# Batch 1's first softmax turned by VectorE and carried to the key partitions through DRAM

## The reference

```python
def sm_attn(qq, kk, vv):
    s = scale * np.matmul(qq, kk.transpose(0, 1, 3, 2))
    s = s - np.max(s, axis=-1, keepdims=True)
    a = np.exp(s)
    a = a / (np.sum(a, axis=-1, keepdims=True) + 1e-09)
    return np.matmul(a, vv)
p_packed = sm_attn(p, k, v)
out = sm_attn(q, p_packed, p_packed)
```

## Time and profile before

| | |
|---|---|
| median of 3 runs | 1526.66 us |
| lowest and highest | 1525.93, 1527.21 us |
| the profiled execution, its own time | 1526.87 us |
| its span | 1525.0 us |
| granted TensorE clock | 1.000 |
| PE busy | 1514.4 us, 99% |
| VectorE, ScalarE, GpSimd busy | 48%, 29%, 13% |

### The profile page before, as it was taken

The page is one execution under the profiler, slowest core; times in us unless marked ns, Lnnn a source line. Parts: engine busy times, 40 slices in busy tenths (PEclk is TensorE's granted clock), DMA queues, the critical chain, the costliest instruction groups (busy, mean ns, idle before and its releaser), DMA issues.

```text
span 1525.0 us, 23354 instructions
## 1 busy us (share of the span) xinstructions
PE 1514.4 (99%) x9430; PEld 1258.7 (83%) x9430; DVE 726.0 (48%) x1234; ACT 444.6 (29%) x789; POOL 192.4 (13%) x197
## 2 busy tenths in 40 slices
PE   8999999999999999999999999999999999999999
PEld 5988888887888888898888888888888888888887
DVE  6675656555564746543343333333333333333333
ACT  4554544534444544422111111111111111111111
POOL 2700000000000000263252020020202001020000
PEclk9999999999999999999999999999999999999999
DMA  9313232130313230233301000010100000010000
GB/s 359 114 41 100 67 99 68 66 100 33 103 36 100 67 98 5 75 131 112 138 1 55 0 28 28 7 49 0 56 0 35 22 28 28 0 55 1 28 0 28
DMA packets 62080, 90.16 MB, mean 59 GB/s; under 512 B 17056, under 2 KB 32416, under 8 KB 61600
## 3 DMA queue, kind: packets, MB, share of 16 engines
q1 hardware_dynamic: 56944, 79.78, 16.4%
q10 hardware_dynamic: 5040, 8.98, 1.5%
HBM read 63.19 MB, written 25.56 MB: 58 GB/s over the span
## 4 chain that ended last, share of the span: by engine, by line
PE 97%; DVE 1%; ACT 0%; DMA 0%; issue 0%; SPq 0%; POOL 0%; DVEq 0%; POOLq 0%
PE psum L735 31%; PE psum L737 30%; PE psum L736 30%; PE psum L931 3%; PE psum L758 1%; PE psum L834 1%; PE psum L807 1%; PE psum L1071 0%; PE psum L863 0%; PE psum L866 0%; PE psum L862 0%; DMA a_keys<-a_mid 0%; PE psum L792 0%; SPq L512 0%; DMA a_mid<-a_rows 0%
## 5 line engine op out<-in xcount | busy, mean ns | idle before, releaser
L1696 DVE TENSOR_TENSOR h_lo<-g,h_hi 128x512 fp32r<-128x512 f32 x144 | 105.8, 735 | 471.0 <-ACT h_hi L1343 471.0
L1343 ACT CAST h_hi<-g 128x512 fp32r<-128x512 f32 x144 | 89.4, 621 | 632.9 <-PE psum L737 600.0
L735 PE MATMUL psum<-an_hi,m_hi 128*128 128x288 f32 x768 | 232.2, 302 | 1.5 <-DVE an_lo L1551 1.2
L736 PE MATMUL psum<-an_hi,m_lo 128*128 128x288 f32 x768 | 225.8, 294 | 0.0
L737 PE MATMUL psum<-an_lo,m_hi 128*128 128x288 f32 x768 | 225.8, 294 | 0.0
L735 PE MATMUL psum<-h_hi,ow_hi 128*128 128x512 f32 (+2 forms) x480 | 182.8, 381 | 0.0
L737 PE MATMUL psum<-h_lo,ow_hi 128*128 128x512 f32 (+2 forms) x480 | 177.6, 370 | 0.0
L736 PE MATMUL psum<-h_hi,ow_lo 128*128 128x512 f32 (+2 forms) x480 | 177.5, 370 | 0.0
L735 PEld LDWEIGHTS psum<-an_hi,m_hi 128*128 128x128 f32 x768 | 144.0, 188 | 24.6 <-issue 14.8
L1652 DVE TENSOR_TENSOR act_sb<-act_sb,psum 128x288 f32<-128x288 f32 x168 | 75.7, 451 | 154.3 <-PE psum L737 136.5
L736 PEld LDWEIGHTS psum<-an_hi,m_lo 128*128 128x128 f32 x768 | 144.3, 188 | 4.2
(11 more groups left out here) (183 smaller groups left out, 2405.0 us busy)
## 6 DMA issues: line engine op xcount, KB each, us to landing
k_sb<-k_t SPq DMA_DIRECT2D x16, 576.0 KB, 5.2
q_sb<-q_t SPq DMA_DIRECT2D x8, 1152.0 KB, 5.5
xs_raw<-y_mid SPq DMA_DIRECT2D x9, 1024.0 KB, 5.2
out_t<-o_sb ACTq DMA_DIRECT2D x34, 256.0 KB, 2.0
gv_sb<-w_gv SPq DMA_DIRECT2D x6, 1024.0 KB, 17.4
w_raw_front<-w SPq DMA_DIRECT2D x10, 512.0 KB, 3.7
v_sb<-v_s SPq DMA_DIRECT2D x12, 320.0 KB, 5.4
a_keys<-a_mid SPq DMA_DIRECT2D x24, 160.0 KB, 3.2
```

The source lines that it names most:

```text
L735: nc.tensor.matmul(dst, w_hi, hi, start=start, stop=False)
L736: nc.tensor.matmul(dst, w_lo, hi, start=False, stop=False)
L1343: nc.scalar.copy(h2_hi[:, f % 2, :], g32[:, f % 2, :]).then_inc(g_hi_done, 1)
L1696: nc.vector.tensor_tensor(h2_lo[:, s, :], g32[:, s, :], h2_hi[:, s, :].bitcast(F32), ALU.subtract).then_inc(g_lo_done, 1)
```

## The change

Batch 1 takes the second way. `turn_keys(1)` on VectorE writes the turned blocks back into a_sb, not into a_rows; SP stores them from there, and its waits for a store of the layer's output and for the Newton steps are left out for batch 1. v of batch 1 is loaded in the order of the key blocks, with four loads. PE's turn_a01 and turn_a2 of batch 1 are gone, and so are the copies on VectorE and ScalarE. The packed products move from the end of block 6 to that of block 7, turn_packed from block 7 to block 8, the tokens from blocks 8 and 9 to 9 and 10, and what follows them on VectorE and ScalarE moves with them; shift1 now stands ahead of block 11's product and gram_lo behind that block. Batch 0 stays on the first way.

```diff
--- before.py
+++ after.py
@@ -83,16 +83,15 @@
 SECOND = {
     "PE": {(0, "ready", 2): ["scores0_ready"], (0, "after", 2): ["scores0"],
            (0, "ready", 3): ["scores1_ready"], (0, "after", 3): ["scores1"],
-           (0, "after", 5): ["turn_a01"], (0, "after", 6): ["turn_a2"], (0, "between", 6): ["packed"],
-           (0, "after", 7): ["turn_packed"],
-           (0, "ready", 8): ["tokens0_ready"], (0, "after", 8): ["tokens0"],
-           (0, "ready", 9): ["tokens1_ready"], (0, "after", 9): ["tokens1"]},
-    "DVE": {(0, "between", 3): ["max0", "max1"], (0, "between", 5): ["turn_a0", "norm0", "norm1"],
-            (0, "after", 6): ["turn_a2"], (0, "within", 7): ["packed"],
-            (0, "after", 8): ["turn_s0", "gram"], (0, "after", 9): ["shift0"], (0, "between", 9): ["turn_s1"],
-            (0, "after", 10): ["gram_lo", "shift1"], (1, "within", 2): ["a2_lo0"]},
+           (0, "between", 7): ["packed"], (0, "after", 8): ["turn_packed"],
+           (0, "ready", 9): ["tokens0_ready"], (0, "after", 9): ["tokens0"],
+           (0, "ready", 10): ["tokens1_ready"], (0, "after", 10): ["tokens1"]},
+    "DVE": {(0, "between", 3): ["max0", "max1"], (0, "between", 4): ["turn_keys"], (0, "between", 5): ["norm0", "norm1"],
+            (0, "within", 8): ["packed"],
+            (0, "after", 9): ["turn_s0", "gram"], (0, "after", 10): ["shift0"], (0, "between", 10): ["turn_s1"],
+            (0, "within", 11): ["shift1"], (0, "between", 11): ["gram_lo"], (1, "within", 2): ["a2_lo0"]},
     "Activation": {(0, "between", 2): ["scores0"], (0, "between", 3): ["scores1"], (0, "after", 4): ["exp0", "exp1"],
-                   (0, "between", 5): ["turn_a1"], (0, "within", 8): ["packed"], (0, "between", 9): ["gram_hi"],
+                   (0, "within", 9): ["packed"], (0, "between", 10): ["gram_hi"],
                    (0, "between", 11): ["probs", "silu"]},
 }
 LATER = {
@@ -348,6 +347,10 @@
 
             return [2 * e + h, 2 + e, 4 + 2 * h + e][min(c, 2)]
 
+        def rows_of_keys(c):
+
+            return a_sb if c == 1 else a_rows
+
         def scores0_of(g):
 
             return psum[:, 2 * g:2 * g + 2, 0:HALF]
@@ -490,7 +493,7 @@
                 sp.dma_start(dst[:], q_t[b].rearrange("(c p) s -> p c s", p=P)).then_inc(q_in, 16)
 
             def load_v(b):
-                if b > 1:
+                if b > 0:
                     for r, (start, n) in enumerate(KEY_BLOCKS):
                         sp.dma_start(v_sb[ROWS * r:ROWS * (r + 1), 0:n, :],
                                      v_s[b][ROWS * start:ROWS * (start + n)].rearrange("(j p) n -> p j n", p=ROWS)).then_inc(v_in, 16)
@@ -502,11 +505,12 @@
 
             def turn_keys(c):
                 for g in range(GROUPS):
-                    sp.wait_ge(rows_turned, GROUPS * (c - 2) + g + 1)
-                    sp.dma_start(a_mid[g], a_rows[:, g, :]).then_inc(rows_out, 16)
-                sp.wait_ge(newton_step, 3 * c + 3)
-                sp.wait_ge(y_stored, 32 * (c - 1))
-                sp.wait_ge(rows_out, 16 * GROUPS * (c - 1))
+                    sp.wait_ge(rows_turned, GROUPS * (c - 1) + g + 1)
+                    sp.dma_start(a_mid[g], rows_of_keys(c)[:, g, :]).then_inc(rows_out, 16)
+                if c > 1:
+                    sp.wait_ge(newton_step, 3 * c + 3)
+                    sp.wait_ge(y_stored, 32 * (c - 1))
+                sp.wait_ge(rows_out, 16 * GROUPS * c)
                 for r, (start, n) in enumerate(KEY_BLOCKS):
                     dst = a_keys[ROWS * r:ROWS * (r + 1)].rearrange("p h j k -> p h (j k)")
                     sp.dma_start(dst, a_mid.rearrange("g (q p) n -> p (g q) n", p=ROWS)
@@ -579,6 +583,7 @@
                     sp.wait_ge(an_lo_done, 2 * BATCH)
                     sp.wait_ge(y_stored, 32 * (BATCH - 1))
                 if b == 0:
+                    turn_keys(1)
                     sp.wait_ge(s2_mm, 4)
                     load_k(2)
                 for f in range(NF1):
@@ -775,12 +780,11 @@
 
             def packed(c):
 
-                if c > 1:
+                if not first(c):
                     packed_of_keys(c)
                     return
-                pe.wait_ge(v_in, 32 * (c + 1))
-                if c == 0:
-                    pe.wait_ge(consts_set, 4)
+                pe.wait_ge(v_in, 32)
+                pe.wait_ge(consts_set, 4)
                 for e in range(2):
                     if e == (1 if first(c) else 0):
                         pe.wait_ge(at_act, c + 1)
@@ -796,10 +800,10 @@
 
             def packed_of_keys(c):
 
-                pe.wait_ge(v_in, 16 * len(KEY_BLOCKS) * c)
+                pe.wait_ge(v_in, 32 + 16 * len(KEY_BLOCKS) * c)
                 pe.wait_ge(mean_copied, 2 * c)
                 pe.wait_ge(m_lo_done, evicted(c))
-                pe.wait_ge(keys_in, 16 * len(KEY_BLOCKS) * (c - 1))
+                pe.wait_ge(keys_in, 16 * len(KEY_BLOCKS) * c)
                 for e in range(2):
                     for j in range(CHUNKS):
                         for pair in range(PAIRS):
@@ -1411,10 +1415,10 @@
             def turn_keys(c):
                 for g in range(GROUPS):
                     dve.wait_ge(exp1_done, GROUPS * c + g + 1)
-                    if g == 0:
+                    if g == 0 and c > 1:
                         dve.wait_ge(an_lo_done, 2 * c)
                         dve.wait_ge(y_stored, 32 * (c - 1))
-                    nc.vector.transpose(a_rows[:, g, :], a_sb[:, g, :]).then_inc(rows_turned, 1)
+                    nc.vector.transpose(rows_of_keys(c)[:, g, :], a_sb[:, g, :]).then_inc(rows_turned, 1)
 
             def packed(c):
                 reached(dve, ppt_mm, c)
```

## The result

The changed kernel takes 1530.44 us (median of 20 runs, 1527.25 to 1531.34), the kernel before 1526.26 (20 runs, 1525.70 to 1527.21). The ratio is 1.0026 with a 95% interval of 1.0020 to 1.0032: slower by 4.2 us, by over 0.2%. Forecast were 1527.2, in a range of 1525.1 to 1528.7. The profiled execution took 1529.91.

What follows compares the result with a forecast made beforehand. PE's matmul stream and its waits were taken as the bound. Terms: -1.10 transposes, +1.43 wait for pp, +0.10 restart, +0.1 silu of block 12, together +0.5 us; forecast 1527.2, range 1525.1 to 1528.7.

Steps and rivals of the forecast that it cites:

- The transposes, 1.10 us: PE's matmul stream loses eight transposes of turn_a01 (0.88) and two of turn_a2 (0.22): 1.10 us gained.
- VectorE's transposes at no cost: VectorE's two added transposes, 1.54 us, end at about 48.2, before PE needs block 5's product: cost nothing.
- The loads of the keys, 4.95 us: Four a_keys loads land 4.95 us after the first issue, 6.2 with slow issues; keys there at 56.1 or 57.3.
- In front of them in SP's queue are the load of v in four pieces rather than two and q's load: SP's queue before the a_mid stores: q lands at 48.9; stores could come 1.5 late, keys 58.8 at worst.
- A late key costs what it is late: PE's packed products: keys up to 57.5 cost nothing more; later ones add what they are past that.
- my sum: PE around block 8: after the keys, packed products 1.45 and the up part 1.57 precede turning pp.
- My own sign of being wrong: PE turning pp without idle time gives 1525.6; products waiting for a_keys past 57.5 give 1527.2 plus the excess.
- The wait for pp decides: PE behind block 8's up part waits 1.4 us for VectorE's pp, which stands behind batch 0's Newton steps and norm.
- The silu of block 12: VectorE's shifted work makes block 11's product, then ScalarE's silu of block 12, late: +0.1 to +0.2 us.
- the second and third rival: Keys late behind q: second, keys at 58.8, 1528.6, chance 0.15; third, stores take 8.9 us, 1532.1, chance 0.05.
- slower by over 0.2%: Whole kernel slower by over 0.2% (3.1 us is 0.2%), through the third rival or something overlooked: chance 0.06.
- The second rival: Stores behind q and slow issues, keys at 58.8, block 8's up part ends 61.9: +1.4, 1528.6; chance 0.15.

Runs made afterwards that it cites:

- e10: Changed kernel (v in four loads of 32 partitions), VectorE's order as in e7, q and p loaded only once the keys landed: 1525.29 us, ratio 0.9994.
- e1: Changed kernel with batch 1's v in the right key order by two loads, of 128 and 64 partitions, instead of four of 32: 1526.53 us, ratio 1.0002.
- e2: Changed kernel with batch 1's v in five loads, four of them of all 128 partitions (wrong key order): 1526.75 us, ratio 1.0003.
- e3: Changed kernel with batch 1's v in two loads of 64 partitions each (wrong key order): 1531.35 us in a single run.
- e11: Changed kernel with batch 1's v in four loads, the first to partitions 32 to 95 (wrong key order): 1527.33 us, ratio 1.0011.
- e4: Changed kernel with eight filler matmuls on TensorE ahead of batch 1's packed products: 1529.02 us, ratio 1.0017.
- e7: Changed kernel with v as in e1 and VectorE scaling batch 1's packed products ahead of batch 0's Newton steps and norm: 1525.97 us, ratio 0.9997.
- e6: Changed kernel, v still in four loads, with q (batch 1) and p (batch 2) loads issued behind the two a_mid stores: 1530.53 us, ratio 1.0023.
- e5: Kernel before the change with batch 1's v in four loads of 32 partitions (wrong key order): 1526.40 us, ratio 1.0000.
- e9: e7 with the loads of q for batch 1 and p for batch 2 issued only once the keys have landed: 1525.54 us, ratio 0.9996.
- e8: e7 with q's load behind the a_mid stores, as in e6: 1530.71 us, ratio 1.0030.

## Why the prediction was wrong

- **The transposes, 1.10 us.** Right. Where the eight stood, L742 starts 0.39 apart (47.64 and 48.03), against 1.27 before (48.08 and 49.35); where the two stood, 0.39 (50.80 and 51.19) against 0.62: 0.88 and 0.23. In e10, where PE waits for neither keys nor pp, 0.7 is left, with 0.2 of it gone in the wait for silu and 0.1 in the restart behind that. The Trainium skill's 275 ns (TensorE: Matmul & The Clock Gate, Part 4: PE-mode transpose) for each, taken as a cost of the stream, would have shown as 2.75; it isn't there.
- **VectorE's transposes at no cost.** Right: they end at 48.00, forecast 48.2. Block 5's product (48.26) stands 0.2 later behind PE's matmuls than before, and PE doesn't wait for it.
- **The loads of the keys, 4.95 us.** Right: 54.44 to 59.39. The 6.2 with slow issues should have been 5.9, since only three quarters of the 1.21 come ahead of the last load; the worst case is then 58.5, and the measured 59.4 is past it all the more.
- **"In front of them in SP's queue are the load of v in four pieces rather than two and q's load; q's is issued at 40.02, and two issues more ahead of it leave SP free long before 47.4. But q lands 8.9 us after its issue".** This is the step that failed. I counted what the four loads cost SP and not what they do to the engines' rate, and took q's 8.9 us over unchanged. It became 13.2, the stores came at 54.4 and not at 51.1 (worst 52.6), the keys at 59.4 and not at 56.1 to 57.5 (worst 58.8). e1 and e2 give it back by v's loads alone; there, with q at 8.8 and 9.0, the stores take 4.4 and 3.0, within the forecast's 3.7 and 1.5 more. e3 and e11 show that loads within one half of the partitions do it.
- **A late key costs what it is late.** Wrong: an idle PE of 3.7 us cost another 1.4 to 1.5 by the clock (e4), a term that the sum and the rivals don't have. At the keys' real 59.4 my sum gives 59.4 + 1.45 + 1.57, so pp turned at 62.4; 64.02 was measured. My own sign of being wrong, 1527.2 and what the products are past 57.5, gives 1529.2 for products at 59.5; 1530.44 was measured.
- **The wait for pp decides.** Its mechanism and size were right (1.25 measured in e2, 1.4 forecast; removed by VectorE's order in e7). In the changed kernel it is gone, since the keys came past 57.5, up to which "that wait swallows a late key".
- **The silu of block 12, 0.1 to 0.2.** Right in seven traces: 0.2 of wait in e1, e2 and e7 to e11. There is none in the changed kernel.
- **The rivals.** What happened is the second and third rival's mechanism (keys late, as the stores queue behind q), which had 0.2 between them; "slower by over 0.2%" had 0.06. Neither had the reason, that the change slows q itself. Against them I had held that only the stores' own bytes remain soon after 49, a reading of a rate that the change itself halved. The second rival's 1.4 on top is also a little high: 61.9 against pp's 60.57 is 1.3.

The profiled execution had one stretch at half clock. Of the 20 runs, two show a mean clock of 1.000 (1527.25 and 1528.29), nine 0.999 (median 1529.91) and nine 0.998 (median 1531.12). In the execution profiled for e6, of 0.998, PE was idle for 3.0 us and the clock was at 0.57 over 8 us, so 6.9 us at half, twice as long; it had fallen while PE was still idle (0.88 from 58 to 59, with no matmul):

```profile
58.00:66.00 8.00, 6.55 (x99) 6.39 (x100) 3.08 (x8) 0.82 (x3) 5.44 (x9) 0.57 0.01 3
58.00:59.00 1.00, 0.00 (x0) 0.00 (x0) 0.93 (x3) 0.00 (x0) 0.00 (x0) 0.88 0.04 8
```

So a part of the changed kernel's spread of 4 us, against 1.5 of the kernel before, goes with the clock. It can't be all. By an estimate from the kernel before's 1526.26, the 3.86 of waiting less the 1.10 of the transposes gives 1529.0 with no half clock at all, and 1527.25 lies 1.8 below that. So the wait for the keys must be shorter in such a run; no trace of one shows it.

## What to carry to other kernels

When an edit reshapes a load, price the bytes a microsecond it will come at, not only its issues, and follow every DMA queued behind it to the one that somebody waits for. A new chain of small DMAs should have no slow large load ahead of it and no large load just behind it; let that load wait for the chain's landing if its own user is far off. The load ahead at its full rate cost the stores here nothing to 1.5 us. Where a wait of some microseconds may fall on TensorE, count its clock too, here 1.4 us on 3.7.

## What the runs showed of the hardware that I had not expected

- A load whose partitions all lie in 0 to 63 or in 64 to 127 came at about half the rate, with the engines as busy: 132 to 193 GB/s in the two stretches from 40 to 43 us (changed kernel, e3, e4, e5, e6, e10), against 335 to 380 (kernel before, e1, e2, e7). 64 partitions across the middle came at 353 (e11).
- Stores of 576 KB took 2.9 us with no load beside them (e9, e10), 4.5 and 4.9 with a load of 1152 KB issued 1 us behind them in the same queue (e6, e8).
- After 3.7 us of idle time TensorE took up work at the full clock and fell to half some 0.2 us later, for 3.4 us; after 3.2 us in e8 it fell 0.6 us after the work began, also for 3.4. In e6 and e3, with 3.0 and 3.5 us idle, it fell while PE was still idle, at 58.8 and 58.7, and stayed at half for 6.8 to 6.9 us. So the longer idle time didn't bring the longer time at half. After 1.25 us (e2) and 1.5 us (e11) it stayed at full.
